# An attention and two-layer kernel: key maxima taken a round ahead, tail projections behind the keys', and x_hi products first where layer 2 begins

## The chip, the cores and the metric

The kernel runs on one core of a Trainium2 chip. The metric is the device time of one execution in microseconds (us), lower is better. The engines are TensorE (PE; PEld are its weight loads), VectorE (DVE), ScalarE (ACT), GpSimd (POOL) and SyncE (SP), which here only issues DMA transfers.

## What is computed

The reference is linear attention with random features for 32 heads (batch 4, 8 heads, 576 tokens, 64 columns, 128 features), followed by two gated layers over 2304 tokens. All is fp32. Cut to what matters:

```python
def phi(x):                       # q and k, each scaled by 64 ** -0.25
    h = x @ omega.T - (x * x).sum(-1, keepdims=True) / 2
    return np.exp(h - h.max(-1, keepdims=True)) / np.sqrt(m)
kv, z = phi(k).T @ v, phi(k).sum(0)
attn = (phi(q) @ kv) / (phi(q) @ z + 1e-6)
x = attn.transpose(0, 2, 1, 3).reshape(2304, 512)
h = x @ w_in;  x = (h * np.clip(h + 3, 0, 6) / 6) @ w_out      # layer 1
h = x @ w_in2; out = (h / (1 + np.exp(-1.702 * h))) @ w_out2   # layer 2
```

## The kernel before

The heads are handled in 16 pairs. 576 tokens are four tiles of 128 and a tail of 64, and the tails of a pair's two heads share one tile. Pairs 0 to 4 (LEAD = 5) come first; the later pairs are spread over the slots of layer 1. A pair goes through these steps, each named after its function, with the engine that does it:

- `projection(a, "q" | "k" | "tail")`, TensorE: the products with omega, into two banks for the queries, two for the keys and one for the tails (L482, and L475 for the tails).
- `maxima`, `norms`, `biases` (together `statistics`), VectorE: the row maximum (L864, L861 for the tails), then h_max and bias (L879, L882), small instructions that need the maximum and half the squared norm of each row. The norms come from squares by ScalarE (`square_rows`, L671), from pair 2 on summed by GpSimd (`fold_rows`, L397 and L399, five halving steps and a last one).
- `exps`, ScalarE: the exponentials, eight instructions for the queries, eight for the keys, two for the tails (L690, L684). A projection of the next pair into the same banks waits for them.
- `turn(a, 0 | 1)`, TensorE: transposes of the query features of one head, which `turned_head` on ScalarE copies out of PSUM (L696). Both heads of a pair use one bank from pair 1 on, so the second waits for the first's copy.
- `key_values(a)`, TensorE: the transposed tail, then the sums kv and z (L510 to L519). `keep` on VectorE copies them out (L897, L899); from pair 1 on `take_tails` copies the former pair's tails to X (L946).
- `quotient(a)`, TensorE: numerators and denominators by token (L533, and L536 for the tails). It waits for both copies of `keep`. `quotient(a)` on VectorE adds EPS, takes the reciprocal and multiplies (L922 to L937), tails included, into `xs`; `turn_back(a)` on TensorE transposes the result (L543); `first_high` (ScalarE) and `first_low` (VectorE) split it into x_hi and x_lo.

Each engine works off its list in the order written out in the block of its engine, and waits on semaphores. One turn of the loop over `a in range(LEAD - 2)` is called a round here.

For the layers each operand is split into a high and a low part, and a product is done in three: high by high, high weights low, low x (L593, L594, L597). A chunk is 512 tokens, the last of a layer 256, and has 16 blocks. `hidden(n)` makes block n of the hidden layer for four k, `gate`, `gated_block`, `high` and `low` make its gated parts, `output(n)` adds it into four banks (L616 to L618). Block n = L2 is the first of layer 2; the first half of its x is split early, the second only when the last block of layer 1 has been gated (`split(c, part=1)`), on ScalarE (x_hi) and VectorE (x_lo).

Of the kernel before, what the change touches and what calls it, by code (L numbers as in the profile page):

```python
# [7 lines left out]
ALU = mybir.AluOpType  # L8
# [3 lines left out]
P = 128  # L12
D = 64
# [14 lines left out]
def build(nc, q_t, k_t, q_n, k_n, v_n, v_tail, omega_t, w_in, w_out, w_in2, w_out2, out):  # L28
# [24 lines left out]
    with ctx:  # L53
# [74 lines left out]
        xs_ready = sem("xs_ready")  # L128
        xs_turned = sem("xs_turned")
# [326 lines left out]
        def _(pe):  # L456
            def projection(a, u):

                pe.wait_ge(load_cols[in_set_b(a)][KQ if u == "q" else KK], 16 * loads_in_set(a))
                if a == LEAD - 1 and u == "tail":  # L460
                    pe.wait_ge(xs_ready, LEAD - 1)
# [61 lines left out]
            def quotient(a):  # L523
# [7 lines left out]
                for h in range(2):  # L531
# [41 lines left out]

            def hidden(n, blocks_k=range(KC)):
                c, s, t = n // J, n % J, size(n)
# [13 lines left out]
                for k in blocks_k:  # L589
# [44 lines left out]
            projection(1, "k")  # L634
            for a in range(LEAD - 2):
                key_values(a)
                projection(a + 1, "tail")
# [3 lines left out]
                projection(a + 2, "k")  # L641
                turn(a + 1, 1)
# [24 lines left out]
        def _(act):  # L667
# [121 lines left out]
            square_rows(1, KQ)  # L789
            turned_head(0, 0)  # L790
            turned_head(0, 1)
            square_rows(1, KK)
            square_rows(2, KQ)
            square_rows(2, KK)
            exps_of(1, "q")
            for a in range(LEAD - 2):
                exps_of(a + 1, "k")
                turned_head(a + 1, 0)
                exps_of(a + 1, "tail")
# [6 lines left out]
                exps_of(a + 2, "q")  # L806
            turned_head(LEAD - 1, 0)
            first_high(LEAD - 2)
            turned_head(LEAD - 1, 1)
            for n in range(2 * L2):  # L810
# [23 lines left out]
                if n == 0:  # L834
                    exps_of(LEAD - 1, "k")
                    exps_of(LEAD - 1, "tail")
# [11 lines left out]
        def _(dve):  # L848
# [55 lines left out]

            def tail_of(h):

                at = ST * (D + 1) + h * (D + 1)
                return slice(h * D, (h + 1) * D), slice(at, at + D), slice(at + D, at + D + 1)

            def quotient(a):  # L910

                tiles = [num_bank(a, h)[:, 0:ST * (D + 1)].rearrange("p (t c) -> p t c", t=ST) for h in range(2)]
                dens_at = (slice(0, ST), slice(ST + 1, GROUPS))
                tails = slice(ST, ST + 1)
                parts = ((0,), (1,)) if a == LEAD - 2 else ((0, 1),)
                for i, heads in enumerate(parts):
                    for h in heads:
                        dve.wait_ge(nd_done, 4 * a + 2 * h + 2)
                        if h == 0:
                            for side in range(2):  # L920
                                rows_h, _, den = tail_of(side)
                                nc.vector.tensor_scalar(dens[rows_h, tails], num_bank(a, 0)[rows_h, den], EPS, None, ALU.add)  # L922
                        last = nc.vector.tensor_scalar(dens[:, dens_at[h]], tiles[h][:, :, D], EPS, None, ALU.add)
                    last.then_inc(dens_set, 1)
                    dve.wait_ge(dens_set, a + i + 1)
                    d = dens[:, 0 if 0 in heads else ST + 1:ST + 1 if 1 not in heads else GROUPS]
# [4 lines left out]
                    for h in heads:  # L931
                        if h == 0:
# [4 lines left out]
                        last = nc.vector.tensor_tensor(xs[:, 0:ST, h * D:(h + 1) * D], tiles[h][:, :, 0:D],  # L937
                                                       dens[:, dens_at[h]].unsqueeze(2).to_broadcast([P, ST, D]), ALU.mult)
                last.then_inc(xs_ready, 1)

# [73 lines left out]
            statistics(0, "tail")  # L1014
# [105 lines left out]
```

## Time and profile before

| | |
|---|---|
| median of 3 runs | 944.45 us (943.81 to 944.54) |
| profiled execution, its own time | 943.76 us |
| its span in the trace | 941.3 us |
| TensorE busy | 932.8 us, 99% |
| VectorE, ScalarE, GpSimd busy | 394.3, 380.5, 169.9 us |
| granted TensorE clock | full in every slice |
| first block of the layers' hidden part issued | 43.79 us |
| first block of layer 2 issued | 541.70 us |

TensorE's products are pipelined, so that a row's duration overlaps with the next row's; what a step costs on TensorE is read from start to start. Idle time in brackets at a row's end is the time before it in which the engine did nothing, with what released it.

### The profile page before, as it was taken

The page shows a single profiled execution, that of the slowest core. Times are in us where ns is not written, and L with a number is a line of the kernel's source. Part 1 is how long each engine was busy: PE and PEld are TensorE (multiplying, and loading weights), DVE is VectorE, ACT ScalarE, POOL GpSimd, SP SyncE. Part 2 cuts the span into 40 slices and gives each one's busy share as a digit, 9 for nine tenths or more (in the row PEclk, how much of TensorE's full clock was granted, in tenths as well). Part 3 has the DMA queues.
Part 4 walks back from the last instruction along what each step waited for, and adds up shares of the span by engine and source line. Part 5 has one row for each costly group of instructions (what it writes and reads, how often), then busy time and mean ns, then how long its engine had stood idle before and what let it go on. Part 6 is the DMA issues. An engine that isn't in the chain of part 4 may idle for free.

```text
span 941.3 us, 12974 instructions
## 1 busy us (share of the span) xinstructions
PE 932.8 (99%) x5126; PEld 782.8 (83%) x5126; DVE 394.3 (42%) x735; ACT 380.5 (40%) x871; POOL 169.9 (18%) x182
## 2 busy tenths in 40 slices
PE   8999999999999999999999999999999999999998
PEld 7878878887888778888889988888888888888898
DVE  6755565555546554452233432232223222422322
ACT  7765655545445444432225642232223222322322
POOL 3656554212221210000006820000000000000000
PEclk9999999999999999999999999999999999999999
DMA  8534341211122110010003600000001000100000
GB/s 276 179 92 145 95 142 27 63 50 52 26 63 64 38 51 13 1 46 1 1 0 107 179 30 1 1 12 34 0 1 46 1 1 0 45 1 1 10 36 24
DMA packets 40731, 45.99 MB, mean 49 GB/s; under 512 B 21600, under 2 KB 22240, under 8 KB 40672
## 3 DMA queue, kind: packets, MB, share of 16 engines
q1 hardware_dynamic: 40304, 44.54, 15.7%
q8 instruction: 41, 0.67, 0.3%
q10 hardware_dynamic: 368, 0.62, 0.2%
q14 instruction: 18, 0.15, 0.0%
HBM read 40.44 MB, written 4.72 MB: 48 GB/s over the span
## 4 chain that ended last, share of the span: by engine, by line
PE 96%; DVE 2%; ACT 2%; issue 0%; DVEq 0%
PE acc L616 14%; PE acc L617 14%; PE acc L618 14%; PE hid L593 11%; PE hid L597 10%; PE hid L594 10%; PE att L593 4%; PE att L594 4%; PE att L597 4%; PE att L519 3%; PE att L482 3%; PE att L561 2%; PE att L504 1%; PE att L475 1%; DVE row_max L864 1%; PE acc L482 0%
## 5 line engine op out<-in xcount | busy, mean ns | idle before, releaser
L616 PE MATMUL acc<-g_hi,w_out_hi 128*128 128x512 f32 (+1 forms) x640 | 241.5, 377 | 0.1
L618 PE MATMUL acc<-g_hi,w_out_lo 128*128 128x512 f32 (+1 forms) x640 | 236.2, 369 | 0.0
L617 PE MATMUL acc<-g_lo,w_out_hi 128*128 128x512 f32 (+1 forms) x640 | 236.0, 369 | 0.0
L593 PE MATMUL hid<-x_hi,w_in_hi 128*128 128x512 f32 (+1 forms) x476 | 181.6, 381 | 0.0
L597 PE MATMUL hid<-x_lo,w_in_hi 128*128 128x512 f32 (+1 forms) x476 | 176.0, 370 | 0.4 <-DVE x_lo L974 0.4
L594 PE MATMUL hid<-x_hi,w_in_lo 128*128 128x512 f32 (+1 forms) x476 | 175.4, 369 | 0.0
L989 DVE TENSOR_TENSOR g_lo<-R,g_hi 128x512 fp32r<-128x512 f32 (+1 forms) x160 | 108.0, 675 | 92.4 <-ACT g_hi L762 92.4
L616 PEld LDWEIGHTS acc<-g_hi,w_out_hi 128*128 128x128 f32 x640 | 120.7, 189 | 21.8 <-issue 2.4
L618 PEld LDWEIGHTS acc<-g_hi,w_out_lo 128*128 128x128 f32 x640 | 120.7, 189 | 20.6
L617 PEld LDWEIGHTS acc<-g_lo,w_out_hi 128*128 128x128 f32 x640 | 120.8, 189 | 19.4
L762 ACT ACTIVATE g_hi<-R 128x512 fp32r<-128x512 f32 (+1 forms) x160 | 94.6, 591 | 84.3 <-DVE R L984 52.6
L593 PEld LDWEIGHTS hid<-x_hi,w_in_hi 128*128 128x128 f32 x476 | 89.8, 189 | 17.1 <-issue 0.2
L982 DVE SCALAR_TENSOR_TENSOR R<-R,hid 128x512 f32<-128x512 f32 (+1 forms) x79 | 49.9, 631 | 129.2 <-ACT R L753 129.2
L597 PEld LDWEIGHTS hid<-x_lo,w_in_hi 128*128 128x128 f32 x476 | 89.6, 188 | 16.2 <-DVE x_lo L974 0.9
L594 PEld LDWEIGHTS hid<-x_hi,w_in_lo 128*128 128x128 f32 x476 | 89.9, 189 | 14.2
L753 ACT ACTIVATE R<-hid 128x512 f32<-128x512 f32 (+1 forms) x79 | 43.9, 556 | 105.8 <-PE hid L597 105.7
L984 DVE TENSOR_TENSOR R<-R,hid 128x512 f32<-128x512 f32 (+1 forms) x40 | 25.4, 634 | 113.5 <-ACT R L755 113.5
L984 DVE TENSOR_TENSOR R<-R,att 128x512 f32<-128x512 f32 (+1 forms) x40 | 25.4, 635 | 113.0 <-ACT R L755 113.0
L755 ACT ACTIVATE R<-att 128x512 f32<-128x512 f32 (+1 forms) x40 | 22.2, 555 | 116.9 <-PE att L597 116.4
L755 ACT ACTIVATE R<-hid 128x512 f32<-128x512 f32 (+1 forms) x40 | 22.2, 555 | 116.3 <-PE hid L597 116.3
L957 DVE RECIPROCAL k_phi<-k_phi 128x288 f32<-128x288 f32 x24 | 46.8, 1949 | 38.6 <-ACT k_phi L708 38.6
L593 PE MATMUL att<-x_hi,w_in_hi 128*128 128x512 f32 (+1 forms) x164 | 60.4, 368 | 0.0
(143 smaller groups left out, 1042.3 us busy)
## 6 DMA issues: line engine op xcount, KB each, us to landing
X<-w_in SPq DMA_DIRECT2D x16, 256.0 KB, 2.7
X<-w_out SPq DMA_DIRECT2D x16, 256.0 KB, 3.2
out_t<-X SPq DMA_DIRECT2D x16, 256.0 KB, 2.3
q_cols<-q_t SPq DMA_DIRECT2D x14, 288.0 KB, 2.9
k_cols<-k_t SPq DMA_DIRECT2D x14, 288.0 KB, 3.6
rows<-q_n SPq DMA_DIRECT2D x13, 288.0 KB, 3.5
rows<-k_n SPq DMA_DIRECT2D x13, 288.0 KB, 3.2
v_rows<-v_n SPq DMA_DIRECT2D x14, 256.0 KB, 3.3
```

The source lines that it names most:

```text
L593: nc.tensor.matmul(bank, w_hi[0][:, at], x_hi[:, k, x0:x0 + t], start=(k == 0), stop=False)
L594: nc.tensor.matmul(bank, w_lo[0][:, at], x_hi[:, k, x0:x0 + t], start=False, stop=False)
L597: last = nc.tensor.matmul(bank, w_hi[0][:, at], x_lo[:, k, x0:x0 + t], start=False, stop=(k == KC - 1))
L616: nc.tensor.matmul(bank, w_hi[1][:, at], g_hi[:, g, 0:t], start=(s == 0), stop=False)
L617: nc.tensor.matmul(bank, w_hi[1][:, at], g_lo[:, g, 0:t], start=False, stop=False)
L618: last = nc.tensor.matmul(bank, w_lo[1][:, at], g_hi[:, g, 0:t], start=False, stop=(s == J - 1))
L755: nc.scalar.activation(R[:, 0:t], h, ACT.Sigmoid, scale=1.702).then_inc(gate_ready, 1)
L762: nc.scalar.activation(g_hi[:, n % G_SLOTS, 0:t], R[:, 0:t], ACT.Copy).then_inc(g_hi_ready, 1)
L957: nc.vector.reciprocal(d, d).then_inc(recip_done, 1)
L982: nc.vector.scalar_tensor_tensor(out=r, in0=r, scalar=6.0, in1=h, op0=ALU.min, op1=ALU.mult).then_inc(gated, 1)
L984: nc.vector.tensor_tensor(r, r, h, ALU.mult).then_inc(gated, 1)
L989: nc.vector.tensor_tensor(g_lo[:, n % G_SLOTS, 0:t], R[:, 0:t], g_hi[:, n % G_SLOTS, 0:t].bitcast(F32), ALU.subtract).then_inc(g_ready, 1)
```

## The change

Five things change, all in the order of work; nothing of the arithmetic is left out.

- The tail of pair a + 2 is projected right behind its keys, not behind the sums of the next pair; pair 1's tail comes ahead of pair 0's sums. The last of the first pairs, pair 4, keeps its late place.
- VectorE takes the maxima of the keys of pair a + 2 in round a, ahead of `first_low(a)`; in the next round only the two small bias instructions are left behind the copies. For pair 1 one of the two maxima is taken ahead of `keep(0)`, and one behind it.
- The tail product L536 comes behind both heads' products, into the second bank. VectorE multiplies the tails last, and reports them by a semaphore of their own, `xs_tails_ready`; `turn_back` no longer waits for them.
- The two first transposes (pair 0) are copied by VectorE (`first_turned`), not by ScalarE; ScalarE takes the exponentials of the tail right behind the keys', ahead of the copy of the turned queries, and those of pair 4's keys ahead of its turns.
- In block L2 the eight products with x_hi come first, then the four with x_lo.

The core of the diff:

```diff
@@ key_values (TensorE)
                 pe.wait_ge(exp_done, 5 * a + 5)
+                if 0 < a < LEAD:
+                    pe.wait_ge(xs_tails_ready, a)
                 nc.tensor.transpose(bank[:, 0:P], tile_of(a, KQ, 0, ST), ident[:])
                 if 0 < a < LEAD:
-                    pe.wait_ge(xs_ready, a)
                     nc.tensor.transpose(old_tails(a), xs[:, ST, :], ident[:])
@@ quotient (TensorE)
-                    if h == 0:
-                        last = nc.tensor.matmul(num_bank(a, 0)[:, ST * (D + 1):(ST + 2) * (D + 1)], tile_of(a, KQ, 0, ST), sums,
+                    if h == 1:
+                        last = nc.tensor.matmul(num_bank(a, 1)[:, ST * (D + 1):(ST + 2) * (D + 1)], tile_of(a, KQ, 0, ST), sums,
                                                 start=True, stop=True)
@@ hidden (TensorE)
-                    if s == 0:
-                        pe.wait_ge(x_ready, x_highs_to(c, k))
-                    last = nc.tensor.matmul(bank, w_hi[0][:, at], x_lo[:, k, x0:x0 + t], start=False, stop=(k == KC - 1))
+                    if n != L2:
+                        last = low_product(n, k)
+                for k in range(KC) if n == L2 else ():
+                    last = low_product(n, k)
@@ order of the first pairs (TensorE)
             projection(1, "k")
+            projection(1, "tail")
             for a in range(LEAD - 2):
                 key_values(a)
-                projection(a + 1, "tail")
                 quotient(a)
                 turn(a + 1, 0)
                 projection(a + 2, "q")
                 projection(a + 2, "k")
+                if a + 2 < LEAD - 1:
+                    projection(a + 2, "tail")
                 turn(a + 1, 1)
                 turn_back(a)
@@ order of the first pairs (ScalarE)
-            square_rows(1, KQ)
-            turned_head(0, 0)
-            turned_head(0, 1)
-            square_rows(1, KK)
-            square_rows(2, KQ)
-            square_rows(2, KK)
+            for a in (1, 2):
+                square_rows(a, KQ)
+                square_rows(a, KK)
             exps_of(1, "q")
             for a in range(LEAD - 2):
                 exps_of(a + 1, "k")
+                exps_of(a + 1, "tail")
                 turned_head(a + 1, 0)
-                exps_of(a + 1, "tail")
                 turned_head(a + 1, 1)
...
+            exps_of(LEAD - 1, "k")
             turned_head(LEAD - 1, 0)
             first_high(LEAD - 2)
             turned_head(LEAD - 1, 1)
@@ quotient (VectorE), its end; turn_back waits for xs_ready
                     for h in heads:
-                        if h == 0:
-                            for side in range(2):
-                                rows_h, num, _ = tail_of(side)
-                                nc.vector.tensor_tensor(xs[rows_h, ST, side * D:(side + 1) * D], num_bank(a, 0)[rows_h, num],
-                                                        dens[rows_h, tails].to_broadcast([D, D]), ALU.mult)
...
                 last.then_inc(xs_ready, 1)
+                for side in range(2):
+                    rows_h, num, _ = tail_of(side)
+                    last = nc.vector.tensor_tensor(xs[rows_h, ST, side * D:(side + 1) * D], num_bank(a, 1)[rows_h, num],
+                                                   dens[rows_h, tails].to_broadcast([D, D]), ALU.mult)
+                last.then_inc(xs_tails_ready, 1)
@@ order of the first pairs (VectorE)
             statistics(0, "tail")
+            first_turned(0)
             maxima(1, "q")
+            first_turned(1)
             norms(1, KQ)
             biases(1, "q")
-            maxima(1, "k")
+            norms(1, KK)
+            dve.wait_ge(proj_done, units_to(1, "k"))
+            maximum(1, "k", 0)
             keep(0)
-            norms(1, KK)
+            maximum(1, "k", 1)
             biases(1, "k")
             for a in range(LEAD - 2):
                 if a > 0:
                     keep(a)
                     take_tails(a - 1)
-                    statistics(a + 1, "k")
+                    biases(a + 1, "k")
                 statistics(a + 1, "tail")
                 quotient(a)
                 statistics(a + 2, "q")
+                maxima(a + 2, "k")
                 first_low(a)
```

How the order stands on the engines that wait or are waited for. TensorE, from the last sums of pair 1 (L519) to its turn_back (L543), before; `hid<-omega` is the tail projection, `acc<-omega` those of queries and keys:

```order
L519 MATMUL att<-v_rows_b,k_phi_b 128x65 x8
L475 MATMUL hid<-omega,q_cols 64x128 x2
L475 MATMUL hid<-omega,k_cols 64x128 x2
L533 MATMUL att<-state,q_phi_b 128x65 x4
L536 MATMUL att<-state,q_tail_phi_b 128x130
L533 MATMUL att<-state,q_phi_b 128x65 x4
L504 MATMUL att<-ident,q_phi 128x128 x4
L482 MATMUL acc<-omega,X 128x128 x16
L504 MATMUL att<-ident,q_phi 128x128 x4
L543 MATMUL att<-ident,x_by_token 128x128 x4
```

The same stretch in the changed kernel:

```order
L521 MATMUL att<-v_rows_b,k_phi_b 128x65 x8
L535 MATMUL att<-state,q_phi_b 128x65 x8
L538 MATMUL att<-state,q_tail_phi_b 128x130
L505 MATMUL att<-ident,q_phi 128x128 x4
L483 MATMUL acc<-omega,X 128x128 x16
L476 MATMUL hid<-omega,X 64x128 x4
L505 MATMUL att<-ident,q_phi 128x128 x4
L545 MATMUL att<-ident,x_by_token 128x128 x4
```

The tail projection (now pair 3's) has moved from between the sums and the quotient to behind the keys' projection, and the quotient follows the sums directly.

VectorE, from the copy of the sums of pair 1 (`keep`) to the first instruction of its quotient, before:

```order
L897 COPY state<-att 128x130
L899 COPY q_tail_phi_b<-att 128x128
L946 COPY X<-att 64x64 x2
L864 TENSOR_REDUCE row_max<-acc 128x4 x2
L879 SCALAR_TENSOR_TENSOR h_max<-row_max,half_norm 128x8
L882 SCALAR_TENSOR_TENSOR bias<-h_max,half_norm 128x8
L861 TENSOR_REDUCE row_max<-hid 128x2
L879 SCALAR_TENSOR_TENSOR h_max<-row_max,half_norm 128x2
L882 SCALAR_TENSOR_TENSOR bias<-h_max,half_norm 128x2
L922 TENSOR_SCALAR dens<-att 64x1 x2
```

And in the changed kernel:

```order
L907 COPY state<-att 128x130
L909 COPY q_tail_phi_b<-att 128x128
L960 COPY X<-att 64x64 x2
L889 SCALAR_TENSOR_TENSOR h_max<-row_max,half_norm 128x8
L892 SCALAR_TENSOR_TENSOR bias<-h_max,half_norm 128x8
L871 TENSOR_REDUCE row_max<-hid 128x2
L889 SCALAR_TENSOR_TENSOR h_max<-row_max,half_norm 128x2
L892 SCALAR_TENSOR_TENSOR bias<-h_max,half_norm 128x2
L937 TENSOR_SCALAR dens<-att 128x4
```

Between the copies and the bias of the keys the two maxima over the keys' banks (L864) are gone; they stand in the round before, ahead of x_lo.

TensorE, the first block of layer 2 and what follows, in the changed kernel (in before each pair of x_hi products was followed by one x_lo product, L593, L594, L597, four times):

```order
L603 MATMUL hid<-x_hi,w_in_hi 128x512
L604 MATMUL hid<-x_hi,w_in_lo 128x512
L603 MATMUL hid<-x_hi,w_in_hi 128x512
L604 MATMUL hid<-x_hi,w_in_lo 128x512
L603 MATMUL hid<-x_hi,w_in_hi 128x512
L604 MATMUL hid<-x_hi,w_in_lo 128x512
L603 MATMUL hid<-x_hi,w_in_hi 128x512
L604 MATMUL hid<-x_hi,w_in_lo 128x512
L580 MATMUL hid<-x_lo,w_in_hi 128x512 x4
L627 MATMUL acc<-g_hi,w_out_hi 128x256
```

The four x_lo products now follow the last x_hi product.

## Rows read from the trace of the kernel before

**Rows 1.** The page: busy time of each engine.
```profile
PE 932.8 (99%) x5126; PEld 782.8 (83%) x5126; DVE 394.3 (42%) x735; ACT 380.5 (40%) x871; POOL 169.9 (18%) x182
```

**Rows 2.** Waits of TensorE (PE), whole span: total us, times, longest.
```profile
PE acc L482 <- ACT k_phi L690: 1.3, 2, 0.8
...
PE acc L482 <- ACT k_phi_b L690: 1.0, 2, 0.8
```

**Rows 3.** Timeline, PE, first pairs: start us, us, what, idle before and releaser.
```profile
13.77 0.33 PE L510 MATMUL att<-ident,q_tail_phi 128*128 128x128 f32 x1
...
16.68 1.08 PE L533 MATMUL att<-state,q_phi 128*128 128x65 f32 x8
...
22.61 0.27 PE L510 MATMUL att<-ident,q_tail_phi_b 128*128 128x128 f32 x1
...
24.88 0.43 PE L475 MATMUL hid<-omega,q_cols 64*64 64x128 f32 x4
...
25.58 1.08 PE L533 MATMUL att<-state,q_phi_b 128*128 128x65 f32 x8
...
27.61 0.61 PE L504 MATMUL att<-ident,q_phi 128*128 128x128 f32 x4
28.15 1.16 PE L482 MATMUL acc<-omega,X 64*128 64x128 f32 x16
30.10 1.16 PE L482 MATMUL acc<-omega,X 64*128 64x128 f32 x16 [0.79 <-ACT k_phi L690]
31.20 0.65 PE L504 MATMUL att<-ident,q_phi 128*128 128x128 f32 x4
...
32.12 0.27 PE L510 MATMUL att<-ident,q_tail_phi 128*128 128x128 f32 x1
...
48.46 0.66 PE L543 MATMUL att<-ident,x_by_token 128*128 128x128 f32 x4 [0.51 <-DVE x_by_token L937]
...
49.48 0.44 PE L475 MATMUL att<-omega,q_cols 64*64 64x128 f32 x4
...
50.06 0.50 PE L593 MATMUL hid<-x_hi,w_in_hi 128*128 128x512 f32 x1
```

**Rows 4.** Timeline, ScalarE (ACT), round of pair 1 and after.
```profile
27.78 2.18 ACT L690 ACTIVATE k_phi<-acc,bias 128x128 f32<-128x128 f32 x8 [1.11 <-DVE bias L882]
...
31.89 0.60 ACT L696 ACTIVATE q_phi<-att 128x512 f32<-128x512 f32 x1 [0.92 <-PE att L504]
...
34.01 2.18 ACT L690 ACTIVATE q_phi_b<-acc,bias 128x128 f32<-128x128 f32 x8
```

**Rows 5.** Timeline, VectorE (DVE), first pairs.
```profile
17.28 0.55 DVE L879 SCALAR_TENSOR_TENSOR h_max<-row_max,half_norm 128x8 f32<-128x8 f32 x1
...
25.89 1.29 DVE L864 TENSOR_REDUCE row_max<-acc 128x4 f32<-128x512 f32 x2
...
46.00 0.32 DVE L922 TENSOR_SCALAR dens<-att 64x1 f32<-64x1 f32 x2 [1.11 <-PE att L536]
...
46.76 0.46 DVE L935 TENSOR_TENSOR x_by_token<-att,dens 64x64 f32<-64x64 f32 x2
...
47.98 0.42 DVE L937 TENSOR_TENSOR x_by_token<-att,dens 128x256 f32<-128x256 f32 x1
```

**Rows 6.** Timeline, PE, where layer 2 begins (541.70) and the block after it.
```profile
541.70 0.40 PE L593 MATMUL hid<-x_hi,w_in_hi 128*128 128x512 f32 x1
541.94 0.40 PE L594 MATMUL hid<-x_hi,w_in_lo 128*128 128x512 f32 x1
542.75 0.50 PE L597 MATMUL hid<-x_lo,w_in_hi 128*128 128x512 f32 x1 [0.42 <-DVE x_lo L974]
...
545.16 0.28 PE L616 MATMUL acc<-g_hi,w_out_hi 128*128 128x256 f32 x1
```

**Rows 7.** Timeline, VectorE, same place.
```profile
541.22 2.48 DVE L974 TENSOR_TENSOR x_lo<-X,x_hi 128x256 fp32r<-128x256 f32 x4
```

**Rows 8.** Timeline, GpSimd (POOL), first fold step.
```profile
16.39 1.41 POOL L397 TENSOR_TENSOR rows<-rows 128x576 f32<-128x576 f32 x1 [14.92 <-ACT rows L671]
```

More of the change, by code:

```diff
@@ L128, in build @@
         xs_ready = sem("xs_ready")
+        xs_tails_ready = sem("xs_tails_ready")
         xs_turned = sem("xs_turned")
@@ L460, in projection @@
                 if a == LEAD - 1 and u == "tail":
-                    pe.wait_ge(xs_ready, LEAD - 1)
+                    pe.wait_ge(xs_tails_ready, LEAD - 1)
                 elif a >= LEAD and u == "tail":
@@ L572, in attend, with low_product @@
                     numerator(a, int(what == "nd1"))
+            def low_product(n, k):
+                c, s, t, x0 = n // J, n % J, size(n), x_columns(n // J)[0]
+                if s == 0:
+                    pe.wait_ge(x_ready, x_highs_to(c, k))
+                return nc.tensor.matmul(hid_bank(n)[:, 0:t], w_hi[0][:, s * 512 + k * P:s * 512 + (k + 1) * P],
+                                        x_lo[:, k, x0:x0 + t], start=False, stop=(k == KC - 1))
             def hidden(n, blocks_k=range(KC)):
@@ L834, in _ @@
                 if n == 0:
-                    exps_of(LEAD - 1, "k")
                     exps_of(LEAD - 1, "tail")
@@ L903, in keep, with first_turned @@
                 nc.vector.tensor_copy(q_turned(a)[:, :, ST * P:S], bank[:, 0:P].rearrange("p (h s) -> p h s", h=2)).then_inc(tails_out, 1)
+            def first_turned(h):
+                dve.wait_ge(turned, h + 1)
+                nc.vector.tensor_copy(q_turned(0)[:, h, 0:ST * P], turn_bank(0, h)[:, 0:ST * P]).then_inc(turned_out, 1)
             def tail_of(h):
-                at = ST * (D + 1) + h * (D + 1)
+                at = (ST + h) * (D + 1)
                 return slice(h * D, (h + 1) * D), slice(at, at + D), slice(at + D, at + D + 1)
@@ L912, in quotient @@
                 tiles = [num_bank(a, h)[:, 0:ST * (D + 1)].rearrange("p (t c) -> p t c", t=ST) for h in range(2)]
-                dens_at = (slice(0, ST), slice(ST + 1, GROUPS))
-                tails = slice(ST, ST + 1)
+                tails = slice(2 * ST, GROUPS)
                 parts = ((0,), (1,)) if a == LEAD - 2 else ((0, 1),)
@@ L918, in quotient @@
                         dve.wait_ge(nd_done, 4 * a + 2 * h + 2)
-                        if h == 0:
+                        if h == 1:
                             for side in range(2):
                                 rows_h, _, den = tail_of(side)
-                                nc.vector.tensor_scalar(dens[rows_h, tails], num_bank(a, 0)[rows_h, den], EPS, None, ALU.add)
-                        last = nc.vector.tensor_scalar(dens[:, dens_at[h]], tiles[h][:, :, D], EPS, None, ALU.add)
+                                nc.vector.tensor_scalar(dens[rows_h, tails], num_bank(a, 1)[rows_h, den], EPS, None, ALU.add)
+                        last = nc.vector.tensor_scalar(dens[:, h * ST:(h + 1) * ST], tiles[h][:, :, D], EPS, None, ALU.add)
                     last.then_inc(dens_set, 1)
                     dve.wait_ge(dens_set, a + i + 1)
-                    d = dens[:, 0 if 0 in heads else ST + 1:ST + 1 if 1 not in heads else GROUPS]
+                    d = dens[:, 0 if 0 in heads else ST:GROUPS if 1 in heads else ST]
                     nc.vector.reciprocal(d, d).then_inc(dens_ready, 1)
@@ L1032, in _ @@
             take_tails(LEAD - 3)
+            biases(LEAD - 1, "k")
             quotient(LEAD - 2)
             first_low(LEAD - 2)
-            statistics(LEAD - 1, "k")
             for n in range(2 * L2):
```

3 lines of the change are left out of this document (1 added, 2 removed).

## Prediction

> **What bounds the kernel now.** I read the busy times first, then TensorE's waits, then the timelines of the first 55 us and of the place where layer 2 begins. TensorE is busy for 932.8 us [rows 1]; its waits, not the other engines' load, are what an order of instructions can change. The reader is to see how few waits there are: the key projection (L482) waits for the exponentials of the keys of the pair before, 1.3 and 1.0 us in four waits [rows 2]; turn_back of pair 3 waits 0.51 us for the quotient, at 48.46 [rows 3]; and the first x_lo product of layer 2 waits 0.42 us [rows 6]. The change aims at these three places. So the sum is made on TensorE alone, stretch by stretch, and for the other engines I ask only whether they deliver in time.
>
> **One round before.** From key_values of pair 1 to that of pair 2, in starts [rows 3]: keys and values 22.61 to 24.88 (2.27); the tail projection of pair 2 then fills the time until the quotient may start, 24.88 to 25.58 (0.70), since the quotient needs VectorE's copies of the sums; quotient 2.03 (to 27.61); turn 0.54; query projection 28.15 to 30.10, of which 0.79 is the wait for the keys; key projection 1.10 (to 31.20); turn and turn_back 0.92 (to 32.12). Together 9.51 us. The round of pair 2 repeats it.
>
> **The change part by part.**
>
> Tails projected behind the keys. A tail projection costs 0.58 us between neighbours that don't wait (49.48 to 50.06 [rows 3]); after the key projection it takes that much. But where it stood it cost nothing: the quotient starts when the copies are there, so the 0.70 us between the end of the keys' sums and the quotient stays, now as an empty gap. Three tail projections (pairs 1, 2, 3) move from a covered place to an uncovered one: 3 x 0.58 = +1.74 us. The work that hid them is VectorE's copy, which is still on the path.
>
> Key maxima a round ahead. In before VectorE took the keys' maxima behind the copies of the sums: maxima start at 25.89 [rows 5], ScalarE's key exponentials start at 27.78 [rows 4], 1.89 later, of which the maxima are 1.29. With the maxima done before, 0.60 is left, so the exponentials may start 1.01 + 0.60 = 1.61 us after the sums end at 24.88 (before: 2.90). The key projection followed the start of these exponentials by 2.32 (27.78 to 30.10). Ready at 1.61 + 2.32 = 3.93; TensorE comes to it at 0.70 + 2.03 + 0.54 + 1.10 = 4.37. No wait by this path, with 0.44 to spare. The other path into the same exponentials is ScalarE's own queue: the turn starts at 31.20 and the query exponentials behind it at 34.01, 2.81 later [rows 3, 4]; then at most 2.18 for them and 2.32 as above, 7.31. TensorE takes 0.92 + 2.27 + 4.37 = 7.56 from that turn to the key projection. Spare: 0.25. The two waits of 0.79 go.
>
> So a new round is 2.27 + 0.70 + 2.03 + 0.54 + 1.10 + 1.10 + 0.58 + 0.92 = 9.24 us, and 8.66 without a tail (the round of pair 2, whose successor's tail stays at its late place).
>
> The start. Key_values of pair 0 stood at 13.77; now the tail of pair 1 is ahead of it, 14.35. Its quotient follows 2.91 later (13.77 to 16.68 [rows 3]), 17.26. Then 2.03 + 0.54 + 1.10 + 1.10 + 0.58 + 0.92: key_values of pair 1 at 23.53, against 22.61, 0.92 late. Here the keys' bias waits for the copies (about 0.6 after 16.56), one maximum (0.65) and the 0.60: exponentials at 18.4, ready at 20.7, wanted at 20.93. Spare only 0.2.
>
> Then 9.24: 32.77 against 32.12. Then 8.66: 41.43, against 41.63 in before (32.12 + 9.51). At this point the attention part has gained 0.2 us: two rounds shorter, but the tails' cover given away.
>
> First transposes copied by VectorE. The trace has no such copy on VectorE. Bounds: 0.60 us, ScalarE's copy of the same tile [rows 4], and 1.29 us, two maxima over 512 columns [rows 5]. I take 0.65, the price of one such maximum, which reads the same tile form. Two of them come where VectorE waited for the squares in before, and ScalarE reaches the query exponentials of pair 1 two copies sooner. TensorE waits for neither. At 0.65 it is worth nothing; at 1.29 each the copies of pair 0's sums come up to 0.7 late, and so does all behind them.
>
> The tails' quotient apart, and pair 4's keys before its turns. TensorE reaches turn_back of pair 3 at 48.46 - 0.51 = 47.95, now 47.75. Pair 3's quotient now has the tails in the second half. It starts 2.97 behind key_values (41.43), at 44.40, and its products are all issued 2.03 later, at 46.43; the last one's end I put 0.2 behind that, an estimate from products that last 0.27 to 0.4 and start 0.1 to 0.2 apart. In before the second half's work was held up behind the first's, which began at 46.00 with the tails [rows 5]. From the tails' denominators to the reciprocal's end is 46.00 to 46.76, 0.76 [rows 5]; the multiplication to TensorE's start is 47.98 to 48.46, 0.48. In sum 46.63 + 1.24 = 47.87. Turn_back starts there instead of at 48.46: -0.59 us in all so far, the 0.2 above within it. The tails' two multiplications (46.76, 0.46 us) leave this path and are done well before the tail projection of pair 4, 1.0 behind turn_back. The key exponentials of pair 4 go into a stretch where ScalarE waited, and are off the later path to the first gate, where TensorE is busy anyway: zero.
>
> Layer 2. Products come 0.24 apart (541.70 to 541.94), 12 of them to the next block: 541.70 + 12 x 0.23 to 0.24 = 544.46 to 544.58. It came at 545.16 [rows 6]. With eight x_hi products first, x_lo is wanted from 543.55 on; VectorE has written the first by 542.7 and all four by 541.22 + 2.48 = 543.70 [rows 7], the fourth being wanted at 544.2. The wait goes with its after-effect: -0.58 to -0.70, I take -0.70, since the usual spacing over many products is 0.23.
>
> **Sum.** -0.59 - 0.70 = -1.29 us. The profiled execution took 943.76 us (span 941.3), so it would be 942.5; against the median of 944.45 it is 943.2. This kernel's runs can tell about 0.2% (1.9 us) from no change, so I forecast no measurable change, a little under before.
>
> **A rule of the Trainium skill.** VectorE's h_max at 17.28 took 0.55 us for eight elements a partition [rows 5] and ended at 17.83; GpSimd's first fold step ran from 16.39 for 1.41, to 17.80 [rows 8]. The Trainium skill, "SBUF — State Buffer", "Who interferes with whom", says that a VectorE instruction with two SBUF inputs and a GpSimd instruction that reads SBUF exclude each other, and the later one waits for the other's whole length. The trace agrees with that rule. It speaks against the change, since the keys' h_max may now fall into the folds of a later pair in each round; what that would cost is rival 1, worked out from rows.
>
> **Rivals.**
> 1. The keys' bias is caught by GpSimd. Mechanism: in each of three rounds h_max stands behind a fold step of up to 1.41 us. For it: the row at 17.28. Against it: ScalarE is the later path in two of the rounds, and the folds now start at another time. Full price: 3 x 1.41 less the spare 0.2 + 0.4 + 0.4 = +3.2, so -1.29 + 3.2 = +1.9: 946.4. It decides, slower than before, once the three delays beyond the spare exceed 1.3 us in sum. Chance 0.08; only its full price, under half of that chance, is more than 0.2%.
> 2. Tails cost nothing. If their small products slipped between others, or the gap of 0.70 shrank with TensorE waiting at the door, 1.74 of cost falls away: -3.0, 941.4. Against it: 0.58 us at 49.48 with nothing waited for. Chance 0.09.
> 3. The layer-2 part does nothing, since the x_lo products still wait at the end or the first gate of the layer, for which ScalarE may not be free so early, passes the wait on: -0.59 only, 943.9. Chance 0.08.
> 4. The key waits stay as they are, the next exponentials being late in ScalarE's queue: about 1.6 of the gain gone, +0.3, 944.8. Chance 0.10.
>
> **The numbers.** The forecast has 0.65 of the chance, with a range of its own of 942.5 to 943.8. For 8 in 10 I reach to rivals 3 and 4 above and half way to rival 2 below: 942.2 to 944.6. Faster by over 0.2% means under 942.6: rival 2 and the low edge of the forecast, 0.15. Slower by over 0.2%: rival 1 at its full price and mishaps in the start, 0.05. No measurable change: 0.80.
>
> **What would show it.** Right: TensorE empty for about 0.6 us behind each key_values of pairs 0, 1, 2; L482 without a wait for k_phi from pair 2 on; rounds of 9.2 and 8.7 us; turn_back of pair 3 near 47.9; twelve products of layer 2's first block in 2.8 us. Wrong: a wait of the key or query projection for exponentials, with h_max over 0.5 us ahead of it; a quotient starting later than 0.7 behind the sums; a tail projection that takes under 0.4; or a wait at the first gate of layer 2.

## The result: 946.8 us, slower by 0.3%

| | before | after |
|---|---|---|
| median of 8 runs each | 944.43 us (943.81 to 945.11) | 946.84 us (945.15 to 949.76) |
| after / before | | 1.003, 95% interval 1.0021 to 1.0039 |
| profiled execution, its own time; span | 943.76; 941.3 us | 947.64; 944.8 us |
| mean granted TensorE clock of its span | 1.000 | 0.995 |
| first block of layer 2 issued | 541.70 us | 545.95 us |

The changed kernel is slower, and outside the range of 942.2 to 944.6. The page answers to [rows 1] with one line, and has a second that was full in before:

```profile
PE 936.2 (99%) x5126; PEld 787.0 (83%) x5126; DVE 398.9 (42%) x737; ACT 379.1 (40%) x869; POOL 169.8 (18%) x182
PEclk9899999999999999999999999999999999999999
```

TensorE is busy for 3.4 us more, with the same 5126 instructions: work that takes longer, not waits. The second line says where to look: in the second of 40 slices (23.6 to 47.2 us) the granted clock isn't full.

TensorE's waits, all that the list has (line, what it waited for, total, times, longest), against [rows 2]:

```profile
PE acc L483 <- DMA k_cols<-k_t: 2.1, 1, 2.1
PE att L492 <- DVE state L1016: 1.1, 1, 1.1
PE att L535 <- DVE q_tail_phi L909: 0.9, 1, 0.9
PE att L535 <- DVE state L907: 0.6, 1, 0.6
PE att L535 <- DVE q_tail_phi_b L909: 0.6, 1, 0.6
```

The waits for the keys' exponentials, for the quotient at turn_back and for x_lo are gone, as forecast. The quotient now waits in rounds 0 to 2 (0.63, 0.63, 0.86 us). The first row is the load of the first keys: 2.15 us here, 0.48 in the profiled execution of before. It varies by execution, from no wait that the lists hold to 2.26 us over the profiles of this case, with no pattern by kernel.

TensorE's timeline of the first pairs, where [rows 3] show before (start, length, instruction, idle time ahead and its releaser; a product of the sums or of the quotient is two records):

```profile
7.60 2.08 PE L483 MATMUL acc<-omega,k_cols 64*128 64x128 f32 x16 [2.15 <-DMA k_cols<-k_t]
...
16.14 0.33 PE L513 MATMUL att<-ident,q_tail_phi 128*128 128x128 f32 x1
...
19.06 1.97 PE L535 MATMUL att<-state,q_phi 128*128 128x65 f32 x16 [0.63 <-DVE state L907]
...
25.19 0.27 PE L513 MATMUL att<-ident,q_tail_phi_b 128*128 128x128 f32 x1
...
32.75 0.65 PE L476 MATMUL hid<-omega,X 64*64 64x128 f32 x8
33.34 0.66 PE L505 MATMUL att<-ident,q_phi 128*128 128x128 f32 x4
33.83 0.60 PE L545 MATMUL att<-ident,x_by_token 128*128 128x128 f32 x4
34.27 0.27 PE L513 MATMUL att<-ident,q_tail_phi 128*128 128x128 f32 x1
...
37.47 2.86 PE L535 MATMUL att<-state,q_phi 128*128 128x65 f32 x16 [0.86 <-DVE q_tail_phi L909]
40.13 0.74 PE L538 MATMUL att<-state,q_tail_phi 128*128 128x130 f32 x2
40.66 1.06 PE L505 MATMUL att<-ident,q_phi_b 128*128 128x128 f32 x4
41.65 2.08 PE L483 MATMUL acc<-omega,q_cols 64*128 64x128 f32 x16
...
46.22 0.27 PE L513 MATMUL att<-ident,q_tail_phi_b 128*128 128x128 f32 x1
...
52.72 0.66 PE L545 MATMUL att<-ident,x_by_token 128*128 128x128 f32 x4
```

Rounds are read from L513 to L513: 9.05, 9.08 and 11.95 us, where 9.18, 9.24 and 8.66 were forecast (9.24 comes out at 9.08 mainly since two projections behind each other take 0.99 each, not 1.10). Of the rounds only the third is off, and of its 3.29 us too much just 0.23 is a longer wait: the same 16 records of the quotient that took 1.97 us at 19.06 take 2.86 at 37.47, and the query projection takes 2.08 instead of 1.16. The windows of that stretch (start and end, length, busy times of PE, PEld, DVE, ACT and POOL, then the granted clock PEclk, the DMA share and GB/s):

```profile
34.00:37.50 3.50, 2.64 (x25) 2.53 (x23) 3.45 (x8) 3.47 (x10) 2.11 (x2) 1.00 0.45 150
37.50:38.50 1.00, 1.00 (x9) 1.00 (x9) 0.92 (x3) 0.82 (x4) 0.92 (x2) 0.91 0.00 0
38.50:42.50 4.00, 4.00 (x23) 3.67 (x24) 2.52 (x12) 3.28 (x11) 3.61 (x8) 0.50 0.33 92
42.50:45.00 2.50, 2.50 (x26) 2.50 (x26) 1.52 (x4) 0.00 (x0) 1.45 (x2) 0.50 0.91 240
```

One microsecond into the quotient that followed the gap of 0.86, the clock falls from 2.4 to 1.2 GHz, and stays there for some 7 us in which TensorE is never idle. The sum in spans closes with that. Forecast was 941.3 - 1.29 = 940.0; 944.8 was measured, 4.8 more. Key_values of pair 1 comes 1.66 late (25.19 for 23.53): the products of the first keys begin 1.45 later (7.60, in before 6.15); the clock falls there too, to 0.57 in the mean from 7.5 to 11.5 us, and the work up to the first turn takes 4.66 instead of 3.23, 1.43 more; two waits for exponentials that stand in before's start disappear behind that, 1.09 less; and round 0 is 0.13 shorter than forecast. The next round is 0.16 shorter than forecast; the third is 3.29 longer (11.95 for 8.66); from there nothing is lost (turn_back of pair 3 is 6.50 behind its key_values, forecast 6.44). 1.66 - 0.16 + 3.29 = 4.79.

The late load and the fall right behind it belong to this execution, the fall in the third round to the kernel: the mean clock was below 1 in all 8 timed runs of after, 0.993 to 0.998, and in 66 of the 79 runs of before that stand beside the experiments it is 1.000. An estimate takes from each run's time (1 - clock) x 942: 946.79 - 3.8 = 943.0, 945.15 - 1.9 = 943.3, 949.76 - 6.6 = 943.2, and over all eight 942.7 to 943.8. At a full clock the changed kernel would by this estimate run in about what was forecast, 943.2. The clock is rounded to 0.001, which is 0.5 us, and e2 below, which kept its clock, came out 1.4 higher than that, so the estimate is good to about a microsecond.

Layer 2, against [rows 6]:

```profile
545.95 0.40 PE L603 MATMUL hid<-x_hi,w_in_hi 128*128 128x512 f32 x1
...
547.79 1.07 PE L580 MATMUL hid<-x_lo,w_in_hi 128*128 128x512 f32 x4
548.70 0.28 PE L627 MATMUL acc<-g_hi,w_out_hi 128*128 128x256 f32 x1
```

Twelve products in 2.75 us without a wait, for 3.46 in before: -0.71 us (forecast: -0.70). The gain is kept to the end: from the first block of layer 2 to the end of the span it is 398.9 us, in before 399.6.

VectorE (first two rows) and GpSimd in the round of pair 1:

```profile
32.38 1.29 DVE L874 TENSOR_REDUCE row_max<-acc 128x4 f32<-128x512 f32 x2
33.77 1.20 DVE L889 SCALAR_TENSOR_TENSOR h_max<-row_max,half_norm 128x8 f32<-128x8 f32 x1
```

```profile
33.67 1.28 POOL L418 TENSOR_TENSOR w_out_lo<-X,w_out_hi 128x512 fp32r<-128x512 f32 x1
```

The h_max of eight elements took 1.20 us and ended at 34.97, with GpSimd's row at 34.95; with GpSimd not in its way it takes 0.17. It is the one at 33.77, the queries' of pair 3, not the keys'. (The keys' bias of that pair is caught too, by a fold step: 0.67 us at 37.98, and no wait of TensorE comes of it.) The h_max delays keep of pair 2, and so makes the third gap 0.86 instead of 0.63: 0.23 us. The Trainium skill, "SBUF — State Buffer", "Who interferes with whom", says that a VectorE instruction with two SBUF inputs and a GpSimd instruction that reads SBUF exclude each other; the trace agrees, with both ends within 0.02 us.

### The profile page after: what moved, and what is told of

The parts are those of the page before. It is cut to its first block, busy times and chain, and to the rows that moved or that the text cites. A ratio compares the mean times of both kernels' runs of the same rounds, so it can differ in the third digit from the quotient of the medians.

```text
span 944.8 us, 12978 instructions
## 1 busy us (share of the span) xinstructions
PE 936.2 (99%) x5126; PEld 787.0 (83%) x5126; DVE 398.9 (42%) x737; ACT 379.1 (40%) x869; POOL 169.8 (18%) x182
## 4 chain that ended last, share of the span: by engine, by line
PE 98%; DVE 1%; DMA 1%; issue 0%; SPq 0%; DVEq 0%
PE acc L627 14%; PE acc L629 14%; PE acc L628 14%; PE hid L603 11%; PE hid L580 10%; PE hid L604 10%; PE att L580 4%; PE att L603 4%; PE att L604 4%; PE att L521 3%; PE att L483 3%; PE att L563 2%; PE att L505 1%; PE acc L483 1%; PE att L535 1%; PE att L476 1%
## 5 line engine op out<-in xcount | busy, mean ns | idle before, releaser
L628 PEld LDWEIGHTS acc<-g_lo,w_out_hi 128*128 128x128 f32 x640 | 120.8, 189 | 19.5
L604 PE MATMUL att<-x_hi,w_in_lo 128*128 128x512 f32 (+1 forms) x164 | 60.4, 368 | 0.0
```

Source lines behind the costliest of these rows:

```text
L604: nc.tensor.matmul(bank, w_lo[0][:, at], x_hi[:, k, x0:x0 + t], start=False, stop=False)
L628: nc.tensor.matmul(bank, w_hi[1][:, at], g_lo[:, g, 0:t], start=False, stop=False)
```

## Experiments

The candidates were named one after another. For the fall of the clock: the empty gap behind the sums alone (A); the late load of the start (B); a gap wider than 0.63 us (W); a gap that is followed by the quotient's eight narrow products in a row, without the wide product L538 between the heads (N); the gap's repetition in short rounds that have no other waits between them (R). And, for the lost time as a whole, waits that come of GpSimd holding up VectorE (C). A narrow product has 65 columns, a wide one 130. Each kernel was timed beside before; the ratios are to these runs of before, with their 95% intervals.

**e1: the tail projections back in the gap**, all else as changed.

```diff
@@ TensorE, first pairs (on after)
-            projection(1, "tail")
             for a in range(LEAD - 2):
                 key_values(a)
+                projection(a + 1, "tail")
                 quotient(a)
...
-                if a + 2 < LEAD - 1:
-                    projection(a + 2, "tail")
```

> The changed kernel with one part undone: the tail of the next pair is projected behind the sums again, in the time in which TensorE has to wait for VectorE's copies; all else stays. Theory A (the time was lost to the granted clock, which fell because that time is now empty): mean clock 1.00 in every run, rounds of 8.7 us, and the 1.74 us of the uncovered tails saved too: 941.6, ratio to before 0.997. Theory B (the clock fell because a transfer of the start was late, whatever stands behind the sums): mean clock 0.993 to 0.998 as in the changed kernel, 944 to 946. Theory C (the keys' bias is held up by GpSimd): waits of the key projection, 943 to 944 with a clock of 1.00.

942.68 us (941.94 to 943.93, 11 runs), ratio 0.9981 (0.9972 to 0.999), clock 1.000 in 10 of 11. 4.2 us under after, more than the 1.74 of the three projections: the rest is the clock. The one run below, 0.998, is the profiled one: the first keys came 2.26 us late, the clock was down from about 8 to 11 us and full in all that follows. So a late load (B) can cost 0.002 of the mean clock; it doesn't bring the falls of the rounds with it. The run missed 941.6 because the gap isn't quite filled: the quotient waits 0.28, 0.23 and 0.60 us, since VectorE comes to the copies later than in before, in round 0 behind a maximum of the keys, and in rounds 1 and 2 again with an h_max behind GpSimd:

```profile
33.31 1.01 DVE L887 SCALAR_TENSOR_TENSOR h_max<-row_max,half_norm 128x8 f32<-128x8 f32 x1
```

**e2: the gap filled with work that does nothing** (two identity products, whose bank the quotient overwrites), **and e7: filled in round 2 alone.**

```diff
@@ TensorE, first pairs (on after; in e7 under "if a == 2:")
                 key_values(a)
+                pe.wait_ge(turned_out, 2 * a + 2)
+                for _ in range(2):
+                    nc.tensor.matmul(num_bank(a, 0)[:, 0:P], ident[:], ident[:], start=True, stop=True)
                 quotient(a)
```

> The changed kernel with two products of the identity with itself (128x128 each, about 0.27 us) put behind the sums of pairs 0, 1 and 2, into a bank that the quotient overwrites; they do nothing for the output. Theory A (empty time lets the clock fall): clock 1.00 in every run and 943.2, since the fill costs nothing in an empty gap of 0.6 us. Theory B (a late transfer at the start): as the changed kernel, 946.8, clock 0.993 to 0.998. Theory C (GpSimd holds up VectorE): 946.8 too, or a little more.

> The changed kernel with the two identity products behind the sums of pair 2 alone, where the clock fell in the profile; the gaps behind pairs 0 and 1 stay empty. Theory W: clock 1.00, 943.2 to 944.6, as with all three filled. Theory N: clock 1.00 or not, it doesn't say. Theory R: the clock stays up or falls at another gap.

e2: 944.62 us (943.22 to 945.41, 11 runs), 0.9999 (0.999 to 1.0008), clock 0.999 or 1.000 in all. TensorE does more than in after and ends 2.2 us sooner. That is still 1.4 above the 943.2 expected; the runs spread from 943.2 to 945.4 with the clock at 0.999 or 1.000, and why isn't settled. e7: 947.53 us (944.34 to 949.14, 10 runs), 1.0029 (1.0018 to 1.004), clock 0.995 to 0.998 in 9 of 10. In its profile the clock is lost behind the gaps that stayed open, those of rounds 0 and 1, and is full at the quotient of the filled one:

```profile
19.00:23.00 4.00, 4.00 (x30) 3.67 (x31) 2.46 (x12) 3.11 (x11) 3.68 (x7) 0.57 0.92 264
29.00:36.50 7.50, 7.50 (x57) 6.95 (x57) 4.86 (x18) 3.66 (x13) 5.68 (x9) 0.54 0.58 161
38.00:42.00 4.00, 3.87 (x35) 3.71 (x34) 2.39 (x9) 4.00 (x14) 2.16 (x2) 1.00 0.00 0
```

**e3: block L2 alone, on before**, the last hunk of `hidden` in the diff.

> The kernel before with the layer-2 part alone: in the first block of layer 2 the eight products with x_hi ahead of the four with x_lo. Mine: no wait there, -0.7 us: 943.7. Rival: the wait is passed on to the next block or the first gate of layer 2: 944.4. Clock 1.00 in both.

944.07 us (942.92 to 945.31, 11 runs), 0.9998 (0.9989 to 1.0006). The times can't tell it from before, nor the -0.7 from the rival; its trace has no wait for x_lo.

**e4: the tail projections behind the keys alone, on before.**

```diff
@@ TensorE, first pairs (on before)
             projection(1, "k")
+            projection(1, "tail")
             for a in range(LEAD - 2):
                 key_values(a)
-                projection(a + 1, "tail")
                 quotient(a)
                 turn(a + 1, 0)
                 projection(a + 2, "q")
                 projection(a + 2, "k")
+                if a + 2 < LEAD - 1:
+                    projection(a + 2, "tail")
```

> The kernel before with one part alone: the tails projected behind the keys, so that the time behind the sums is empty and the waits of the key projection are still there. By the schedule alone three uncovered tails, +1.7 us: 946.1. Theory A (empty time behind the sums lets the clock fall): clock below 1.00 in most runs and 948 to 951. Theory B (late transfer at the start): clock 1.00 unless the first transfers are late, 946.1. Theory C: 946.1, clock 1.00.

946.18 us (945.57 to 946.86, 11 runs), 1.0017 (1.0008 to 1.0026). The term of +1.74 stands: 944.4 + 1.74 = 946.1. But the clock is 1.000 in all 11 runs, and theory A falls: three gaps of 0.63 us are there,

```profile
27.15 1.08 PE L533 MATMUL att<-state,q_phi_b 128*128 128x65 f32 x8 [0.63 <-DVE q_tail_phi_b L901]
28.06 0.44 PE L536 MATMUL att<-state,q_tail_phi_b 128*128 128x130 f32 x2
28.34 1.00 PE L533 MATMUL att<-state,q_phi_b 128*128 128x65 f32 x8
```

and this stretch and those around the two other gaps are at full clock.

**e5: the tail product back between the heads**, all else as changed.

```diff
@@ TensorE, quotient (on after); VectorE reads num_bank(a, 0), turn_back waits for xs_tails_ready
-                    if h == 1:
-                        last = nc.tensor.matmul(num_bank(a, 1)[:, ST * (D + 1):(ST + 2) * (D + 1)], tile_of(a, KQ, 0, ST), sums,
+                    if h == 0:
+                        last = nc.tensor.matmul(num_bank(a, 0)[:, ST * (D + 1):(ST + 2) * (D + 1)], tile_of(a, KQ, 0, ST), sums,
```

> The changed kernel with the tail product L536 back behind the first head's products and in the first bank, so that no eight narrow products stand in a row; turn_back then waits for the tails' quotient too (0.46 us for pair 3). Theory W (the clock falls at the gap behind the sums of pair 2, which is 0.86 us wide instead of 0.63, since VectorE's h_max was caught for 1.20 us by GpSimd): clock as in the changed kernel, 0.993 to 0.998, 946.8 to 947.3. Theory N (the stretch of eight narrow products behind the gap is what lets it fall): clock 1.00, 943.6. Theory R (not one gap but their repetition each 9 us, with no other waits between them): as W here.

944.03 us (943.4 to 948.12, 11 runs), 1.0003 (0.9992 to 1.0014); clock 1.000 in 8 runs, 0.995 or 0.996 in 3, which are the three over 946. In the profile a gap of 0.91 us, wider than any in after, is followed by the full clock (1.00 from 35 to 45 us). The three gaps come back in short rounds (9.08, 9.04 and 8.95 us) without a wait for the keys, which by R should have cost the clock. No profile shows the three runs that lost it. The row of the widest gap:

```profile
36.50 1.08 PE L535 MATMUL att<-state,q_phi 128*128 128x65 f32 x8 [0.91 <-DVE q_tail_phi L909]
37.41 0.44 PE L538 MATMUL att<-state,q_tail_phi 128*128 128x130 f32 x2
```

**e6: both maxima ahead of the query bias**, which takes h_max out of GpSimd's way, so that no gap is over 0.63.

```diff
@@ VectorE, first pairs (on after)
-                statistics(a + 2, "q")
+                maxima(a + 2, "q")
                 maxima(a + 2, "k")
+                biases(a + 2, "q")
                 first_low(a)
```

> The changed kernel with one order changed on VectorE: in each round both maxima (queries, keys) first and the queries' h_max and bias behind them, so that h_max stands behind GpSimd's subtraction instead of within it and VectorE is free when the sums of pair 2 are done. Theory W (gap of 0.86): gap 0.63, clock 1.00, 943.2. Theory N (narrow products): clock 0.993 to 0.998, 946.8. Theory R (repetition): also 946.8, clock below 1.00, with all gaps at 0.63.

947.82 us (947.32 to 949.65, 5 runs), 1.0043 (1.0031 to 1.0055), clock 0.993 to 0.995. All three gaps are 0.63 us and the clock is lost more, not less: 0.57 from 19.5 to 23.5 us, 0.54 from 29.5 to 37.0. Theory W falls, and so does C: the queries' h_max takes 0.17 us in rounds 0 and 1 here, every gap is 0.63, and more time is lost than in after.

**e8: the changed kernel again.**

> The changed kernel once more, on this chip and beside the other three. If the lowered clock belongs to the kernel and not to the day: clock 0.993 to 0.998 in nearly all runs, 946.8, and in the trace half the clock from about 37.5 us on for 7 us. If it was an accident of those runs: 943.2, clock 1.00.

946.79 us (945.62 to 949.72, 9 runs), 1.0028 (1.0017 to 1.0039), clock 0.993 to 0.996 in all. Its profiled execution had a wait of only 0.50 us for the first keys, so the start is not what takes the clock (B). It falls at two of the three quotients:

```profile
28.00:32.00 4.00, 4.00 (x33) 3.67 (x33) 2.23 (x11) 2.65 (x10) 3.67 (x7) 0.57 0.71 197
32.00:38.50 6.50, 5.87 (x62) 5.47 (x59) 5.01 (x15) 4.55 (x14) 3.43 (x3) 1.00 0.29 81
38.50:42.50 4.00, 4.00 (x32) 3.67 (x33) 2.48 (x11) 2.93 (x11) 3.60 (x8) 0.57 0.35 90
```

**e9: e4, with the tail product last.** Gap and row of narrow products, in the order of before, with its waits for the keys.

```diff
@@ on e4: TensorE, quotient; VectorE then waits for both heads
-                    if h == 0:
+                    if h == 1:
                         last = nc.tensor.matmul(num_bank(a, 0)[:, ST * (D + 1):(ST + 2) * (D + 1)], tile_of(a, KQ, 0, ST), sums,
@@ VectorE
-                        dve.wait_ge(nd_done, 4 * a + 2 * h + 2)
+                        dve.wait_ge(nd_done, 4 * a + 4)
```

> The kernel before with two parts: the tails projected behind the keys (as in the run with that part alone, which kept its clock at 1.00 and took 946.2), and the tail product L536 behind both heads' products; VectorE then waits for both heads (up to 0.8 us for pair 3). By the schedule 946.2 to 947.0. Theory N (an empty gap followed by eight narrow products lets the clock fall): clock 0.995 to 0.998, 949 to 951. Theory R (it needs the short rounds of the changed kernel, without key waits): clock 1.00, 947.0.

949.82 us (949.24 to 950.39, 5 runs), 1.0061 (1.0048 to 1.0073), clock 0.994 to 0.996 in all. Its rows beside those of e4, same gap, same products, another order:

```profile
28.53 2.50 PE L533 MATMUL att<-state,q_phi_b 128*128 128x65 f32 x16 [0.63 <-DVE q_tail_phi_b L901]
30.82 0.74 PE L536 MATMUL att<-state,q_tail_phi_b 128*128 128x130 f32 x2
```

```profile
29.50:37.00 7.50, 7.50 (x56) 6.77 (x56) 5.34 (x20) 3.29 (x12) 5.34 (x9) 0.54 0.60 171
```

Moving one product of 130 columns by four places costs the clock: 3.6 us over e4, of which some 0.9 is the longer wait at turn_back (1.35 for 0.5 us), since VectorE now begins the quotient later. N stands. R falls here too: the order is that of before, a wait for the keys (0.74 us) stands in round 2, and yet the clock is lost.

**e11: a wide product between the heads again**, added to the changed kernel; L538 stays last.

```diff
@@ TensorE, quotient (on after), behind the four products of a head
+                    if h == 0:
+                        last = nc.tensor.matmul(num_bank(a, 0)[:, ST * (D + 1):(ST + 2) * (D + 1)], tile_of(a, KQ, 0, ST), sums,
+                                                start=True, stop=True)
```

> The changed kernel with one more product of the form of the tail product (128x130) between the two heads' narrow ones, into columns that nothing reads; it adds 0.27 us to each of four quotients, and L536 stays last, the gaps stay empty. Theory N (the row of eight narrow products behind the gap): clock 1.00 in most runs, 943.2 + 1.1 = 944.3. Theory R or any other that leaves the narrow products out: clock 0.993 to 0.998 as in the changed kernel, 947.9.

944.55 us (943.59 to 947.12, 11 runs), 1.0005 (0.9996 to 1.0014), clock 1.000 in 9 of 11 (0.999 and 0.996 once each). More work than after, gaps as open (0.63, 0.63, 0.64), 2.3 us less. N again, by an edit that adds nothing but a product.

**e10: e1 with the order of e6.**

> The changed kernel with the tail projection back behind the sums and with both maxima ahead of the queries' h_max and bias on VectorE, a candidate that may beat both. The quotient waited 0.3, 0.2 and 0.6 us behind the tail projection in the run with the first edit alone (942.7), since GpSimd held h_max for up to 1.0 us; by the order of the second edit h_max stands behind that: waits under 0.2 each, 942.0 to 942.3, clock 1.00. Rival: h_max is caught by another GpSimd step, 942.7.

940.85 us (940.64 to 941.14, 5 runs), 0.9965 (0.9953 to 0.9978), clock 1.000 in all: faster than both kernels, and by over 1 us more than expected. Its waits list holds three entries, none of the quotient's; h_max takes 0.17:

```profile
PE acc L483 <- DMA k_cols<-k_t: 1.1, 1, 1.1
PE att L492 <- DVE state L1014: 1.1, 1, 1.1
PE acc L483 <- ACT k_phi L701: 0.5, 1, 0.5
```

```profile
32.13 0.17 DVE L887 SCALAR_TENSOR_TENSOR h_max<-row_max,half_norm 128x8 f32<-128x8 f32 x1
```

Its three rounds take 8.52, 8.50 and 8.50 us (L513 at 13.90, 22.42, 30.92, 39.42), e1's 8.68, 8.75 and 9.05: 0.96 of the 1.83 between the medians. Where the rest comes from isn't settled; the starts differ from one execution to the next by as much.

**e12: e1 with pair 0's transposes copied by ScalarE again.**

```diff
@@ ScalarE, start (on e1); VectorE without first_turned
-            for a in (1, 2):
-                square_rows(a, KQ)
-                square_rows(a, KK)
+            square_rows(1, KQ)
+            turned_head(0, 0)
+            turned_head(0, 1)
+            square_rows(1, KK)
+            square_rows(2, KQ)
+            square_rows(2, KK)
```

> The changed kernel with the tail projection back behind the sums (942.7) and the first two transposes copied by ScalarE again. My prediction's step: these copies are worth nothing, 942.7. Rival: ScalarE reaches the query exponentials two copies later, and the key projection of pair 2 waits: up to +0.5, 943.2. Clock 1.00.

943.18 us (942.15 to 946.3, 11 runs), 0.9992 (0.9983 to 1.0), three runs with a clock of 0.996 to 0.998. In its profile the clock is full throughout, though the quotient waits 0.41 us in round 0 and 0.88 in round 1, behind the tail projection and ahead of eight narrow products:

```profile
27.32 1.97 PE L535 MATMUL att<-state,q_phi_b 128*128 128x65 f32 x16 [0.88 <-DVE q_tail_phi_b L910]
```

So an idle stretch ahead of the eight narrow products isn't enough. In every kernel that regularly lost the clock it also follows directly on the sums; whether the tail projection helps by shortening the idle time or by its own products isn't shown. The median is 0.5 over e1's, less than either's scatter. What the copies on VectorE are worth, between nothing and half a microsecond, stays open.

## Why the prediction was wrong

The step that failed is how the sum joins two steps of the change: "so the 0.70 us between the end of the keys' sums and the quotient stays, now as an empty gap", priced as 3 x 0.58 for the work that left it, and the tail product behind both heads, priced by its effect on turn_back alone. The first price is right when the step stands alone (e4: 946.2 for 946.1). What the two do together to the clock of the products that follow was put at nothing, without a word on it: every term was worked out at the full clock that before shows, and no rival was for the granted clock. Measured in its place: 3.29 us more than forecast in the third round of the profile, all but 0.23 of it from products that run at half the clock, and 2 to 7 us a run by the mean clocks. The runs side by side:

| kernel | gap behind the sums | eight narrow products in a row | clock below 0.999 | median us |
|---|---|---|---|---|
| before | filled | no | 8 of 79 runs | 944.2 to 944.4 |
| e3 | filled | no | 3 of 11 | 944.1 |
| e4 | empty | no | 0 of 11 | 946.2 |
| e5 | empty | no | 3 of 11 | 944.0 |
| e11 | empty | no | 1 of 11 | 944.6 |
| e1 | 0.28, 0.23, 0.60 left | yes | 1 of 11 | 942.7 |
| e12 | 0.41, 0.88, 0 left | yes | 3 of 11 | 943.2 |
| e2 | 0, 0, 0.37 left | yes | 0 of 11 | 944.6 |
| e10 | filled | yes | 0 of 5 | 940.9 |
| after, e8 | empty | yes | 17 of 17 | 946.8 |
| e6 | empty | yes | 5 of 5 | 947.8 |
| e7 | two of three empty | yes | 9 of 10 | 947.5 |
| e9 | empty | yes | 5 of 5 | 949.8 |

Neither edit alone takes the clock as a rule, though single runs lose it with either or none (e5 down to 0.995, before to 0.996). Both together take it in 36 of 37 runs. What it costs: some 4 us at 0.57, or 7 to 7.5 us at 0.50 to 0.54, once or twice an execution, 2 to 7 us in all by the clocks. That it is these two edits is shown by taking each away and by putting both into before. How the chip comes to its decision isn't: the nine falls in the rounds of the profiles all begin within a quotient, behind one or two of the three like places, not always the same ones, and e1 and e12 have gaps of 0.60 and 0.88 ahead of eight narrow products at full clock. What tells these apart stays open.

The other steps:

- One round: forecast 9.18 and 9.24 us, measured 9.05 and 9.08; the third is seen without the clock's loss in e5, 8.95 for 8.66, of which 0.28 is its gap of 0.91 instead of 0.63. Right, at a full clock.
- Tails: 0.58 each, 0.59 at 32.75; e4 confirms the sum. Rival 2 is out.
- Key maxima: no wait for the keys' exponentials from pair 2 on. Rival 4 is out.
- GpSimd: the catch cost something in one round alone, 0.23 us, on the queries' h_max. The mechanism of rival 1 was right in kind, its victim and its size of 3.2 us were not.
- Turn_back of pair 3: no wait, 6.50 behind its key_values for a forecast of 6.44. Right.
- Layer 2: -0.71 in the trace, kept to the end of the span. Rival 3 is out by the trace; the times of e3 alone don't decide it.
- VectorE's copies of the first transposes took 0.68 and 0.69 us (taken: 0.65), nearer to the maximum than to the upper bound of 1.29.

So the schedule's sum of -1.29 held to about a microsecond, which is as far as these runs can tell, and the sign came out wrong by a resource that the sum did not have in it. Writing down what the change does to TensorE's stretch behind each set of sums, an idle 0.6 us and then eight products of 65 columns, would have raised the question; before's trace, at full clock in every slice, had no row to price it from.

## What to carry to other kernels

An empty gap on a busy TensorE has two prices, its length and what it does to the clock of the work behind it; look at the clock column before and after, in every run, and take a rise of TensorE's busy time at an equal count of instructions as the sign. Where a gap can't be avoided, try work in it or a wide product among the narrow ones that follow: here the one saved 2.2 us (e2) and the other 2.3 (e11), with more work in both. Of an order with several edits, time each alone and in pairs: the tails behind the keys cost 1.7 us alone (e4) and 5.4 with the tail product last (e9), and the change without the gap, its maxima in another order (e10), runs 0.35% under before.

## What the hardware did that I had not expected

- Gaps of 0.63 us sufficed, given the narrow products behind them (e6, e8, e9). The Trainium skill, "TensorE: Matmul & The Clock Gate", "A second HAM failure mode: psum-queue depth-cycling", tells of a kernel in which the engine idles for very short times between groups of products and moves between both levels for it; the trace agrees in kind. The Trainium skill, same page, "HAM oscillation — how this bites in real kernels", puts the falls of another kernel down to its waits for transfers; that isn't the cause in the rounds here, where the wait is for two copies by VectorE and lasts 0.63 us.
- While the clock was down in the rounds TensorE was busy without a break (4.00 of 4.00, 7.50 of 7.50 us in e7), and it still took some 4 to 7.5 us to come back.
- At the start, a wait of 2.15 (after) or 2.26 us (e1) for the first keys was also followed by a fall of the clock, between 7.5 and 11.5 us; waits of 1.44 (e5) and 1.10 us (e10) weren't. These waits vary by execution. That they make a good part of the scatter of before's own runs is likely but not shown: before has one profile.
